# Routing rows to their experts inside the SoLU tiles instead of in a stage of its own

## The chip, the cores and the metric

One core of a Trainium2 chip runs the whole program. The time is device microseconds of one execution, median of three runs. Engines: PE (TensorE; PEld is its weight loading), ACT (ScalarE), DVE (VectorE), POOL (GpSimd), SP (SyncE, which here only issues DMAs). Each engine runs its own instructions in order; they meet at semaphores. A DMA that SP or POOL issues is carried by the core's 16 DMA engines.

## The reference, cut to what matters

```python
attn = masked_attention(q, k, v, centroids)       # 16 heads, 768 rows, head size 64
x = attn as (1536, 512)
h = x @ w_in                                      # (1536, 1024)
solu = h * softmax(h); ln = layer_norm(solu) * g_ln
x = ln @ w_out                                    # (1536, 512): the rows that are routed
logits = x @ w_gate                               # 8 experts
expert = argmax(logits); gate_w = softmax(logits)[expert]
for i in range(1536):                             # in order of the rows
    if counts[expert[i]] < 384: pos[i] = counts[expert[i]]; counts[expert[i]] += 1
out[i] = gate_w[i] * (relu(x[i] @ w1[e]) @ w2[e]) # e = expert[i]; 0 where a row found no place
```

The place of a row is its rank among the rows of the same expert, so it depends on all rows before it.

## The kernel before, in words

Four blocks follow one another, each closed by a barrier of all engines.

**Attention** (`attention`, to about 322 us): 16 heads of 6 query tiles. SP moves the next heads' operands (`load_qk`, `move_hi` with the wait of L279, `move_lo`, `move_mask`, `load_v`), one head after the other, waiting for the engines between them.

**SoLU** (`solu_block`, to about 466 us): 12 tiles of 128 rows, in software-pipelined slots (`tiles_of`). In slot i PE turns ln(i) (`turn_ln`, L129), multiplies tile i+2 into h (`up`, L121), turns x2(i-1) (L950), multiplies tile i down (`down`, L941, 24 matmuls) and multiplies x2(i-1) with the gate (`gate`, L958). ACT copies the high part of the turned ln (L885), cuts x, takes the square root for tile i+1 (L75), copies turned x2 (L878), takes the exponentials of tile i+2 (L70, with its accumulator read) and copies x2(i) out of PSUM (L900). DVE makes the low part (L917), copies the logits (L912), normalises tile i+1 (L92 to L109) and takes the maximum of tile i+2 (L79). SP stores each x2 tile to DRAM (L840). POOL cuts x and, in the first slots, expert 0's weights (L866, L868). The two x2 tiles and one PSUM bank for x2 are used in turn.

**Route** (`route`, 466 to 480 us): on all 1536 rows at once DVE makes one-hot rows, running sums over tiles, softmax weights and places; PE adds up the ranks (L1065 to L1068) and, with 12 matmuls (L1071), turns (place -> row) into `info`, for each of 24 expert tiles the row numbers and weights. DVE packs into `mask` which tiles hold rows.

**Experts** (`experts`): 8 experts with 3 token tiles each. SP loads weight pieces of 512 KB into a ring of 7. POOL gathers a tile's rows by `info` (`gather`, L1246, an indirect DMA) into one of 4 buffers and scatters results into `out` (L1260). In POOL's order gather(g+4) stands ahead of the wait for result g. PE turns the rows (L1403), multiplies up a pair of tiles (L1413), the third tile if `mask` says that it holds rows, and down (L1449).

## Time and profile before

| | us |
|---|---|
| median of 3 runs | 717.92 (714.87 to 720.31) |
| the profiled execution | 717.02 |
| its span | 715.2 |
| PE busy / DVE / ACT / POOL | 636.6 / 432.9 / 397.0 / 294.8 |
| mean granted clock of TensorE | 0.965 of full |

Starts in the timeline count from the start of the span; the execution's own time is 1.8 us above the span. Matmul ends are modelled, so starts are the safer numbers.

### The profile page before, as it was taken

How to read it: one execution, taken by the hardware profiler on the slowest of the kernel's cores; microseconds unless marked ns; L12 is line 12 of the kernel's file. 1: busy time of each engine (PE TensorE's matmuls, PEld its weight loads, DVE VectorE, ACT ScalarE, POOL GpSimd, SP SyncE). 2: the span in 40 equal slices, each digit the busy share in tenths (PEclk: the TensorE clock that was granted, in tenths of full speed). 3: DMA queues.
4: the chain of work that ended last, by engine and by line, in shares of the span. 5: the costliest groups of instructions: out<-in, count | busy, mean ns of one | idle time of the engine just before them, and what ended most of it. 6: DMA issues, size and time to landing. Idle time of an engine off the chain costs nothing. (4 is left out here: it accounts for less than half of the span.)

```text
span 715.2 us, 12775 instructions
## 1 busy us (share of the span) xinstructions
PE 636.6 (89%) x4596; PEld 570.7 (80%) x4596; DVE 432.9 (61%) x788; ACT 397.0 (56%) x671; POOL 294.8 (41%) x277
## 2 busy tenths in 40 slices
PE   2799999999999999789999998726998999999993
PEld 1799989898989899578888887615897988888982
DVE  6588888888888887356646546162563326545620
ACT  3488888887878788345454454202454335444520
POOL 3447676767876857357321000012123030341221
PEclk9999999999999999989999999956999999999997
DMA  5746565545464430073110000008666255666310
GB/s 124 214 113 155 129 159 127 141 113 150 123 163 120 111 90 2 0 245 139 45 47 26 15 30 16 29 20 292 208 210 197 83 182 192 233 206 209 110 35 12
DMA packets 37379, 86.10 MB, mean 120 GB/s; under 512 B 6719, under 2 KB 8895, under 8 KB 37314
## 3 DMA queue, kind: packets, MB, share of 16 engines
q1 hardware_dynamic: 33474, 75.78, 36.0%
q0 software_dynamic: 3840, 9.45, 3.9%
q8 instruction: 42, 0.69, 0.4%
q14 instruction: 23, 0.19, 0.1%
HBM read 53.74 MB, written 12.58 MB: 93 GB/s over the span
## 5 line engine op out<-in xcount | busy, mean ns | idle before, releaser
L557 DVE TENSOR_TENSOR p_lo<-lnt_ps,p_hi 128x384 f16<-128x384 f32 x192 | 104.6, 547 | 29.4 <-ACT p_hi L433 29.3
L433 ACT ACTIVATE p_hi<-lnt_ps 128x384 f16<-128x384 f32 x192 | 91.6, 489 | 50.7 <-PE lnt_ps L675 48.0
L552 DVE TENSOR_REDUCE neg_max<-h_ps 128x1 f32<-128x768 f32 x96 | 91.4, 952 | 20.7 <-PE h_ps L664 20.5
L675 PE MATMUL lnt_ps<-consts,p_exp 128*128 128x128 f32 x576 | 93.1, 277 | 7.6 <-DVE p_lo L557 5.7
L687 PE MATMUL one_ps<-v_cut,p_hi 128*128 128x193 bf16 x576 | 92.0, 248 | 0.7 <-ACT pv_sb L433 0.7
L664 PE MATMUL h_ps<-KK,QQ 128*128 128x384 f32 x384 | 91.9, 362 | 0.0
L1260 POOL DMA_INDIRECT out<-x_t,info x24 | 24.3, 1013 | 160.5 <-ACT x_t L1269 124.8
L688 PE MATMUL one_ps<-v_cut,p_lo 128*128 128x129 bf16 x576 | 89.5, 219 | 0.0
L455 ACT ACTIVATE p_exp<-h_ps,neg_max 128x768 f32<-128x768 f32 x96 | 86.4, 900 | 1.7 <-DVE neg_max L552 1.7
L675 PEld LDWEIGHTS lnt_ps<-consts,p_exp 128*128 128x128 f32 x576 | 69.7, 144 | 19.0 <-issue 12.7
L664 PEld LDWEIGHTS h_ps<-KK,QQ 128*128 128x128 f32 x384 | 63.4, 192 | 0.2 <-issue 0.2
L688 PEld LDWEIGHTS one_ps<-v_cut,p_lo 128*128 128x128 f16 x576 | 56.6, 98 | 1.1
L687 PEld LDWEIGHTS one_ps<-v_cut,p_hi 128*128 128x128 f16 x576 | 55.6, 96 | 1.1 <-DVE p_lo L557 1.1
L917 DVE TENSOR_TENSOR lnt_lo<-lnt_ps,lnt_hi 128x1024 fp32r<-128x1024 f32 x12 | 14.7, 1225 | 58.9 <-ACT lnt_hi L885 58.9
L352 POOL TENSOR_TENSOR qk_lo<-qk,qk_hi 128x768 fp32r<-128x768 f32 x16 | 29.3, 1830 | 49.8 <-ACT qk_hi L433 46.6
L1269 ACT ACTIVATE eht_hi<-eh_ps 128x512 fp32r<-128x512 f32 x32 | 19.2, 599 | 52.2 <-PE eh_ps L1413 48.9
L1359 DVE SCALAR_TENSOR_TENSOR eht_lo<-eh_ps,eht_hi 128x512 fp32r<-128x512 f32 x32 | 22.2, 692 | 37.1 <-ACT eht_hi L1269 34.2
L63 POOL TENSOR_TENSOR xs_lo<-x_t,xs_hi 128x512 fp32r<-128x512 f32 x12 | 15.5, 1292 | 67.0 <-ACT xs_hi L58 67.0
L1246 POOL DMA_INDIRECT x_t<-x_rows,info x24 | 33.0, 1376 | 23.6 <-issue 20.5
L1413 PE MATMUL eh_ps<-xs_hi,w_hi 128*128 128x256 f32 x128 | 37.6, 294 | 3.1 <-issue 1.7
L1269 ACT ACTIVATE x_t<-ey_ps,info 128x512 f32<-128x512 f32 x16 | 11.0, 688 | 52.8 <-PE ey_ps L1449 29.6
L941 PE MATMUL one_ps<-w_out_hi,lnt_hi 128*128 128x512 f32 x96 | 39.5, 411 | 0.0
(225 smaller groups left out, 1676.7 us busy)
## 6 DMA issues: line engine op xcount, KB each, us to landing
w_raw<-in_w SPq DMA_DIRECT2D x40, 512.0 KB, 5.1
x_t<-in_w SPq DMA_DIRECT2D x24, 512.0 KB
QQ<-qk_hi SPq DMA_DIRECT2D x32, 192.0 KB, 3.2
KK<-qk_hi SPq DMA_DIRECT2D x32, 192.0 KB, 3.7
qk<-in_qT SPq DMA_DIRECT2D x16, 192.0 KB, 3.7
qk<-in_kT SPq DMA_DIRECT2D x16, 192.0 KB, 4.4
QQ<-qk_lo SPq DMA_DIRECT2D x16, 192.0 KB, 4.0
KK<-qk_lo SPq DMA_DIRECT2D x16, 192.0 KB, 4.1
```

Source lines behind the costliest of these rows:

```text
L433: return nc.scalar.activation(out, in_, ACT.Copy, **kw)
L455: nc.scalar.activation(as_banks(p_exp[g % PX][:, :]), both(s_ps[g % 2]), ACT.Exp, bias=neg_max[:, g % PB:g % PB + 1]).then_inc(exp_done, 1)
L552: V.tensor_reduce(neg_max[:, g % PB:g % PB + 1], both(s_ps[g % 2]), AX.XY, ALU.max, negate=True).then_inc(max_done, 1)
L557: V.tensor_tensor(p_lo[g % PB][:, TH * i:TH * (i + 1), :], t_ps[i][:, 0:HALF].rearrange("p (k q) -> p k q", q=P), p_hi[g % PB][:, TH * i:T ...
L664: ins = mm(s_ps[g % 2][:, i, 0:HALF], QQ[s][:, j, P * t:P * (t + 1)], KK[s][:, j, HALF * i:HALF * (i + 1)], start=j == 0, stop=j == 1)
L675: ins = nc.tensor.transpose(t_ps[i][:, P * k:P * (k + 1)], p_exp[g % PX][:, P * kt:P * (kt + 1)], ident)
L687: mm(pv_ps[:, 0:VW], p_hi[g % PB][:, kt, :], vc[:, kt, :], start=kt == 0, stop=False)
L688: ins = mm(pv_ps[:, D:VW], p_lo[g % PB][:, kt, :], vc[:, kt, D:VW], start=False, stop=kt == T - 1)
L941: ins = mm(x2_ps[:, :], x[:, c, :], wout[w][:, c, :], start=n == 0, stop=n == 3 * FC - 1)
L1246: nc.gpsimd.indirect_dma_start(x_in[b][:, :], None, x2_dram, bass.IndirectOffsetOnAxis(ap=info[:, g, 0:1].bitcast(U32), axis=0), bounds_ch ...
L1269: return nc.scalar.activation(out, in_, func, **kw)
L1413: ins = mm(h_ps[b][:, width * i:width * (i + 1)], w[wp][:, c, P * f:P * (f + 1)], x(xp, c), start=n == 0, stop=n == 3 * KC - 1)
```

## The change

The `route` block is gone. Its work is done tile by tile in the SoLU slots, with single-tile operands of 128x8 or 128x1: `pick_expert(i-1)` on DVE at the end of slot i, `gate_exps(i-1)` on ACT ahead of the copy of x2(i), `positions(i-2)` on PE behind `turn_ln(i)` (two small bf16 matmuls into the x2 bank, which `down(i)` may not overwrite before DVE has read them), `weight_rows(i-2)` and `place_rows(i-2)` on DVE between L917 and `normalise`. The gate's matmuls stand in the middle of `down`. An x2 tile has two more columns, row number and weight, and POOL scatters its 514-column rows into a DRAM tensor sorted by expert and place (`send`), in place of SP's store. The experts then read tiles and `info` with plain loads that SP issues: four of each ahead of the weights, the later ones between weight pieces. Since unfilled places are read too, SP fills the tensor with empty rows (24 DMAs of 128 rows, two per head) during attention. `mask` is made from the last tile's counts.

```diff
 def attention(...):
+            sp.wait_ge(empty_set, 2)
             for h in range(HEADS):
...
+                for i in range(EMPTY * h, min(EMPTY * (h + 1), SLOT_TILES)):
+                    sp.dma_start(x2_dram[P * i:P * (i + 1), :], empty_row[:, :]).then_inc(filled, 16)
+            sp.wait_ge(filled, 16 * SLOT_TILES)
...
             cut_v(0)
+            Gp.memset(empty_row[:, :], 0.0).then_inc(empty_set, 1)
+            pool.wait_ge(empty_set, 1)
+            Gp.iota(empty_row[:, DM:DM + 1].bitcast(I32), ...).then_inc(empty_set, 1)
 def solu_block(...):
@@ POOL
+            def send(i):
+                s = i % 2
+                pool.wait_ge(x2_out, i + 1)
+                pool.wait_ge(weight_step, 2 * (i + 1))
+                pool.wait_ge(place_step, PLACE * (i + 1))
+                Gp.indirect_dma_start(x2_dram, bass.IndirectOffsetOnAxis(ap=place[s]..., axis=0),
+                                      x2[s][:, :], None, ...).then_inc(stored[s], 16)
+            for i in range(NT):
                 if i >= 3:
                     start.cut_x_low(pool, i, i % 2)
+                if i >= 5:
+                    send(i - 5)
+                if i < PW:
...
+            for i in range(NT - 5, NT):
+                send(i)
+            for s in range(2):
+                pool.wait_ge(stored[s], 16 * (NT // 2))
@@ ACT
+            def gate_exps(i):
+                act.wait_ge(neg_done, i + 1)
+                if not below(i, 1):
+                    act.wait_ge(weight_step, 2 * i)
+                nc.scalar.activation(ex[:, :], lg, ACT.Exp, bias=neg_lg[:, 0:1],
+                                     accum_out=total[:, 0:1]).then_inc(ex_done, 1)
@@ ACT, slot i
                     start.exps(act, i + 2, s, e_sb[:, :, :])
+                if not below(i, 1):
+                    gate_exps(i - 1)
                 act.wait_ge(x2_full, i + 1)
                 if not below(i, 2):
                     act.wait_ge(stored[s], 16 * n)
@@ DVE, six operations: maximum, ranked, best, hot16, neg_lg, base
+            def pick_expert(i): ...
@@ DVE, three operations: row number, total + 1e-9, reciprocal
+            def weight_rows(i, s, n): ...
@@ DVE, five operations
+            def place_rows(i, s):
+                dve.wait_ge(pos_full, i + 1)
+                V.tensor_tensor(mine[:, :], pos_ps, hot16[:, :], ALU.mult).then_inc(pos_read, 1)
+                V.tensor_tensor(before16[:, :], before16[:, :], hot16[:, :], ALU.add)
...
+                V.scalar_tensor_tensor(place[s][:, :], pos[:, :], base[:, 0:1], over[:, :], ALU.add,
+                                       ALU.add).then_inc(place_step, 1)
@@ DVE, slot i
                 if not below(i, 2):
-                    logits_out(i - 2)
+                    weight_rows(i - 2, s, n - 1)
+                    place_rows(i - 2, s)
                 if exists(i + 1):
                     start.normalise(...)
                 if exists(i + 2):
                     start.top(dve, i + 2, s)
+                if not below(i, 1):
+                    pick_expert(i - 1)
@@ PE, down(i)
+                if not below(i, 2):
+                    pe.wait_ge(pos_read, i - 1)
                 for c in range(FC):
+                    if c == FC // 2 and not below(i, 1):
+                        gate(i - 1)
@@ PE, turn_x2(i)
-                    pe.wait_ge(lg_out, i)
+                    pe.wait_ge(hot_done, i)
+                    pe.wait_ge(ex_done, i)
@@ PE
+            def positions(i):
+                pe.wait_ge(hot_done, i + 1)
+                pe.wait_ge(x2_out, i + 2)
...
+                ins = mm(pos_ps, tri16[:, :], hot16[:, :], start=True, stop=False)
+                ins = mm(pos_ps, ones16[:, :], before16[:, :], start=False, stop=True)
+                ins.then_inc(pos_full, 1)
             def slot(i, s, n):
                     start.turn_ln(pe, i, ln)
+                if not below(i, 2):
+                    positions(i - 2)
                 if exists(i + 2):
                     start.up(pe, i + 2, s)
...
-                if not below(i, 1):
-                    gate(i - 1)
             turn_x2(NT - 1, (NT - 1) % 2)
+            positions(NT - 2)
             gate(NT - 1)
+            positions(NT - 1)
-def route(...): ...
 def experts(...):
@@ SP
+            for g in range(XB):
+                load_x(g)
+            for g in range(XB):
+                load_info(g)
             for e in range(1, E):
                 for j in range(PW):
                     n = piece(e, j)
                     if n >= RAW:
                         sp.wait_ge(w_lo, n - RAW + 1)
                     load_expert_piece(...).then_inc(raw_in[n % RAW], 16)
+                    g = CT * e + j - (PW - CT)
+                    if j >= PW - CT and g >= XB:
+                        load_x(g)
+                        load_info(g)
@@ POOL
-            for g in range(XB):
-                gather(g)
...
             for g in range(G):
-                if g + XB < G:
-                    gather(g + XB)
                 b = g % 2
                 pool.wait_ge(y_done, g + 1)
```

## Rows read from the trace of the kernel before

**Rows 1.** Stages: attention, one SoLU slot, the placing stage. Columns in the first row.

```profile
core 0: us, PE busy (x) PEld busy (x) DVE busy (x) ACT busy (x) POOL busy (x), PEclk, DMA share, GB/s
20.00:330.00 310.00, 292.79 (x2574) 269.82 (x2574) 241.49 (x454) 232.86 (x453) 205.90 (x179) 0.99 0.48 129
387.90:401.18 13.28, 13.28 (x71) 11.15 (x70) 7.19 (x16) 6.71 (x9) 1.30 (x1) 1.00 0.05 20
470.00:480.00 10.00, 3.10 (x15) 2.85 (x15) 7.33 (x31) 0.00 (x0) 0.00 (x0) 0.50 0.00 1
```

**Rows 2.** Timeline, one SoLU slot (i=6) and the next one's start: start us, us, what.

```profile
388.22 1.03 ACT L885 ACTIVATE lnt_hi<-lnt_ps 128x1024 fp32r<-128x1024 f32 x1 [1.12 <-PE lnt_ps L129]
...
390.42 0.16 DVE L912 COPY logits<-one_ps 128x8 f32 x1
390.49 0.14 DVE L92 TENSOR_SCALAR den<-den 128x1 f32<-128x1 f32 x1
390.67 0.16 DVE L93 RECIPROCAL den<-den 128x1 f32<-128x1 f32 x1
...
393.84 0.19 PEld L941 LDWEIGHTS one_ps<-w_out_hi,lnt_hi 128*128 128x128 f32 x1
...
394.44 0.22 DVE L104 SCALAR_TENSOR_TENSOR root<-root 128x1 f32<-128x1 f32 x1
...
399.65 0.19 ACT L70 ACTIVATION_READ_ACCUMULATOR e_sb<-h_ps,neg_top 128x1 f32 x1
399.85 0.60 ACT L900 ACTIVATE x<-one_ps 128x512 f32<-128x512 f32 x1
400.27 0.94 PEld L129 LDWEIGHTS lnt_ps<-consts,ln 128*128 128x128 f32 x8
...
401.18 1.00 PEld L121 LDWEIGHTS h_ps<-w_in_hi,xs_hi 128*128 128x128 f32 x5
...
401.49 1.03 ACT L885 ACTIVATE lnt_hi<-lnt_ps 128x1024 fp32r<-128x1024 f32 x1 [1.04 <-PE lnt_ps L129]
```

**Rows 3.** Chain that ended last, from the first gather on: start us, us, what.

```profile
482.67 6.72 DMA x_t<-x_rows,info
...
491.97 12.86 PE eh_ps L1413 x96
```

**Rows 4.** Timeline, expert 2: its third token tile.

```profile
544.96 0.66 PE L1403 MATMUL ext_ps<-consts,x_t 128*128 128x128 f32 x4 [2.60 <-DMA x_t<-x_rows,info]
```

**Rows 5.** Stretches, columns as in rows 1: expert 2's first half.

```profile
541.00:566.00 25.00, 22.40 (x177) 21.80 (x175) 10.25 (x12) 9.05 (x13) 4.52 (x4) 0.93 0.50 162
```

**Rows 6.** SP's waits in attention: us in total, times, longest.

```profile
SPq L279 <- PE h_ps L664: 49.3, 14, 3.5
```

**Rows 7.** Timeline, slot 1: the operation of L104 beside POOL's weight cuts.

```profile
327.71 0.91 DVE L104 SCALAR_TENSOR_TENSOR root<-root 128x1 f32<-128x1 f32 x1
```

**Rows 8.** Timeline, the last two SoLU tiles (10 and 11).

```profile
447.11 0.58 ACT L878 ACTIVATE x2t<-one_ps 128x512 f32<-128x512 f32 x1
...
452.13 0.95 PEld L129 LDWEIGHTS lnt_ps<-consts,ln 128*128 128x128 f32 x8
...
462.20 0.60 ACT L900 ACTIVATE x<-one_ps 128x512 f32<-128x512 f32 x1 [5.01 <-PE one_ps L941]
...
463.28 0.42 PEld L950 LDWEIGHTS one_ps<-consts,x 128*128 128x128 f32 x4 [0.41 <-ACT x L900]
...
465.72 0.17 DVE L912 COPY logits<-one_ps 128x8 f32<-128x8 f32 x1 [2.56 <-PE one_ps L958]
```

**Rows 9.** Timeline, the last scatter of the kernel.

```profile
708.70 0.99 POOL L1260 DMA_INDIRECT out<-x_t,info  x1 [0.30 <-issue]
```

**Rows 10.** DMA issues: SoLU's rows to DRAM, KB each, median us to landing.

```profile
x_rows<-x SPq DMA_DIRECT2D x12, 256.0 KB, 2.0
```

**Rows 11.** Timeline, weight load of the second transpose of expert 0.

```profile
489.44 0.71 PEld L1403 LDWEIGHTS ext_ps<-consts,x_t 128*128 128x128 f32 x4 [0.39 <-DMA x_t<-x_rows,info]
```

**Rows 12.** L1246, the gathers: duration ns min/median/max of 24.

```profile
L1246 POOL DMA_INDIRECT x_t<-x_rows,info x24: 997/1274/2089, 481.1 to 683.3; - x24
```

More of the change, by code:

```diff
@@ L800, in solu_block @@
         lnt_lo = sb("lnt_lo", [P, FC, P], F32R)
-        x2 = [sb(f"x2_{s}", [P, DM], F32) for s in range(2)]
+        x2 = [sb(f"x2_{s}", [P, DM + 2], F32) for s in range(2)]
         x2t = sb("x2t", [P, KC, P], F32)
         zeros = x2[1]
+        number = sb("number", [P, NT], I32)
+        tri16 = sb("tri16", [P, P], BF16)
+        ones16 = sb("ones16", [P, P], BF16)
+        top = sb("r_top", [P, 1], F32)
+        neg_lg = sb("r_neg", [P, 1], F32)
+        ranked = sb("r_ranked", [P, E], F32)
+        best = sb("r_best", [P, 1], F32)
+        base = sb("r_base", [P, 1], F32)
+        hot16 = sb("r_hot16", [P, E], BF16)
+        before16 = sb("r_before16", [P, E], BF16)
+        ex = sb("r_ex", [P, E], F32)
+        total = sb("r_total", [P, 1], F32)
+        mine = sb("r_mine", [P, E], F32)
+        pos = sb("r_pos", [P, 1], F32)
+        over = sb("r_over", [P, 1], F32)
+        place = [sb(f"r_place{s}", [P, 1], I32) for s in range(2)]
+        held = sb("r_held", [1, E, CT], F32)
+        held_sum = sb("r_held_sum", [1, 1], F32)
         lnt_ps = start.lnt_ps
@@ L845, in _ @@
             sp.wait_ge(zeroed, 1)
-            sp.dma_start(x2_dram[NT * P:NT * P + 1, :], zeros[0:1, :]).then_inc(zeros_stored, 16)
             for t in range(NT):
-                sp.dma_start(a["out"][t * P:(t + 1) * P, :], zeros[:, :]).then_inc(zeros_stored, 16)
-            for i in range(PW - RAW):
-                store(i, i % 2)
-                load(i + RAW)
-            with sp.Fori((PW - RAW) // 2, NT // 2) as n:
-                for s in range(2):
-                    store(2 * n + s, s)
@@ L855, in _ @@
-            for s in range(2):
-                sp.wait_ge(stored[s], 16 * (NT // 2))
-            sp.wait_ge(zeros_stored, 16 * (NT + 1))
+                sp.dma_start(a["out"][t * P:(t + 1) * P, :], zeros[:, 0:DM]).then_inc(zeros_stored, 16)
+            for j in range(RAW, PW):
+                load(j)
+            sp.wait_ge(zeros_stored, 16 * NT)
         @block.gpsimd
         def _(pool):
-            nc.gpsimd.memset(zeros[:, :], 0.0).then_inc(zeroed, 1)
-            for i in range(PW):
+            Gp = nc.gpsimd
@@ new lines, in weight_rows @@
+            def weight_rows(i, s, n):
+                if not below(i, 2):
+                    dve.wait_ge(stored[s], 16 * n)
+                if below(i, 1):
+                    dve.wait_ge(constants, 1)
+                V.tensor_copy(x2[s][:, DM:DM + 1].bitcast(I32), number[:, bass.ts(i, 1)])
+                dve.wait_ge(ex_done, i + 1)
+                V.tensor_scalar(total[:, :], total[:, :], 1e-9, None, ALU.add).then_inc(weight_step, 1)
+                dve.wait_ge(weight_step, 2 * i + 1)
+                V.reciprocal(x2[s][:, DM + 1:DM + 2], total[:, :]).then_inc(weight_step, 1)
@@ L946, in turn_x2 @@
                 pe.wait_ge(x2_out, i + 1)
-                if not (isinstance(i, int) and i == 0):
-                    pe.wait_ge(lg_out, i)
+                if not below(i, 1):
+                    pe.wait_ge(hot_done, i)
+                    pe.wait_ge(ex_done, i)
                 for c in range(KC):
@@ L1492, in build @@
         consts = sb("consts", [P, width], F32)
-        logits = sb("logits", [P, NT, E], F32)
         info = sb("info", [P, E * tiles_per_expert, 2], I32)
```

311 lines of the change are left out of this document (115 added, 196 removed).

## The prediction

> **What bounds the kernel now.** I read the stretches first [rows 1]. In attention PE is busy 292.8 of 310 us with the DMA engines at a share of 0.48. In a SoLU slot PE has no idle at all: 13.28 of 13.28 us. In the ten microseconds of placing, PE has 3.1 us of work at a clock of 0.50 of full, the lower level (1.2 GHz), POOL and ACT have none, and DVE does 31 small operations: a serial stretch in which the whole core waits.
>
> Second, the timeline of a slot [rows 2] says how close the other engines are. The slot repeats after 13.27 us (L885 at 388.22 and 401.49). ACT's and DVE's round (L885, L917, normalise, maximum, exponentials, copy of x2) reaches L900 at 399.85 and ends 0.60 later, 12.23 us after it began. Only 1.04 us of it are slack. This is the number on which the SoLU part turns.
>
> Third, the chain that ended last [rows 3] goes from the placing through a gather of 6.72 us to the first matmul of expert 0 at 491.97. The weight loads were issued ahead of that gather. From then on the chain is PE's but for one place: in expert 2 PE waits 2.60 us for the third tile's gather [rows 4], which POOL issues only after a result of the expert before, and the clock then drops, to 0.93 over 25 us [rows 5].
>
> Fourth, SP in attention waits 49.3 us for PE at L279 alone, 3.5 us in each of 14 heads [rows 6].
>
> **Part 1: empty rows in attention.** Added are 24 DMAs of 263 KB, 6.3 MB, two in each of 12 heads, with an issue of some 0.5 us each. Two cost about 1 us of SP against its 3.5 us of waiting per head [rows 6], and the DMA engines are half free [rows 1]; what they delay is loaded a head ahead of its use. At 129 GB/s for a share of 0.48, full engines would carry 269 GB/s, so a fill takes 0.98 us of them. I take +0.5 us for all. Without the cover it would be 24 x 0.98 = 23.5 us; the bounds of what I believe are 0 and 3.
>
> **Part 2: the steady slot.** DVE gets eight operations between L917 and L92 in the place of one (L912). One that depends on nothing starts 0.07 after the one before (390.42, 390.49), one that waits for the last result 0.18 (390.49, 390.67) [rows 2]. Four wait (reciprocal, sum, limit, place), at 0.2; four do not, at 0.07 to 0.1; less the one removed that is +1.0 us. ACT gets a small exponential with its accumulator read: 0.20 from read to next start (399.65, 399.85) [rows 2] and 0.15 for the rest, +0.35. `pick_expert` follows the maximum and lies beside the table load and the exponentials, free. So L900 can start 11.63 + 1.35 = 12.98 us after L885, and its copy ends at 13.58; by itself this round now takes 13.6.
>
> PE gets two matmuls with 8 columns. The trace has none of that size; between 0.07 and 0.4 I take 0.2. The gate only moves. But `positions` stands right behind `turn_ln` and waits for the copy of x2, which cannot end before 1.10 us after the start of `turn_ln` (0.44 until the last matmul is out and seen, 0.60, a signal), while `up` now starts after 0.91 (400.27, 401.18) [rows 2]. The rest of a slot is 13.27 - 0.91 = 12.36. PE's own round becomes 1.10 + 0.2 + 12.36 = 13.66. The two rounds are also joined: from `turn_ln` 1.22 to L885 (400.27, 401.49) [rows 2], 13.58 to the end of the copy, 0.06, 0.2, then 12.36 to the `turn_ln` after next: 27.42 for two slots, 13.71 each. That is +0.44 in each of the eight slots 2 to 9, 3.5 us. Extra DVE time d counts half up to 0.2 and whole beyond. In slots 2 to 4 POOL cuts weights beside it, and there the operation of L104 took 0.91 for 0.22 [rows 2, 7]; half of that 0.69 in three slots is 1.0. Part 2: **+4.5 us**, from 1.6 (matmuls only, 0.2 a slot) to 8 (all eight operations at 0.18 or more).
>
> What is queued behind the new waits: behind PE's in `positions` all of `up`; behind `pos_read` in `down` nothing new, as DVE reads the ranks some 2 us ahead of `down` (393.84) [rows 2]. ACT's wait for the scatter of tile i-2: its place is known some 3.4 us after L885, POOL starts at most 0.9 later and needs 1.0 to 2.1, landing 2.0, so 8.4 at worst, 4.5 us before L900 asks.
>
> **Part 3: the last tiles, the routing's rest, the first rows.** In slot 10 turned x2 is copied at 447.11 [rows 8], behind the square root; DVE's 1.0 shifts that to 448.1, and the gate, now in the middle of `down`, waits for it. Gate 1.0 and twelve matmuls at 0.233 after 448.7 give `turn_ln(11)` at 452.6 for 452.13: +0.5. In slot 11 the gate inside `down` puts 1.0 ahead of the last copy: 463.7 for 462.20. The last transpose no longer waits for the logits' copy (463.28, where the x2 copy had ended at 462.80), so it starts at 464.4, and 2.44 later (463.28 to 465.72) [rows 8] the logits are there: 466.85. Then in series: four operations of DVE 0.8, the negative 0.1, ACT's exponential with signals 0.4, and total, reciprocal, product, sum, limit, place 1.15: 469.3. POOL starts 0.5 later and takes 0.99 [rows 9]: 470.8. The scatter's landing has no row. Plain stores land 2.0 after issue [rows 10]; behind the kernel's last scatter all that follows, landing and closing, takes 715.2 - 709.69 = 5.5. I take 2.0, between 1.0 and 5.5: 472.8. Barrier and first issue 0.5. The first rows' loads now stand ahead of the weights; two of 256 KB, 2.5 and 0.4 (between the 2.0 of [rows 10] and the 6.72 of [rows 3]): 476.2. From the second transpose to the first matmul 2.53 (489.44, 491.97) [rows 3, 11]: 478.75. The mask is made beside the scatter. So expert 0 starts 491.97 - 478.75 = **13.2 us** earlier, before part 2 is added; 5.5 with both DMAs at their upper ends, 15 with both at the lower. PE is cold in both kernels when it begins expert 0, so its 12.86 us stay.
>
> The Trainium skill, "DMA: Bandwidth & Descriptors", section "Anatomy of one DMA — SWDGE (gpsimd) path", gives 2.0 us and bytes over 436 GB/s for a DMA: an estimate of 2.6 us for the scatter and as much for a load. By that expert 0 would start 0.7 us later.
>
> **Part 4: the experts.** 24 gathers leave POOL. SP issues the rows of tile 3e+2 behind the last weight piece of expert e, which needs only that the first piece of e has been cut, early in expert e-1: a lead of most of an expert. So the wait of 2.60 [rows 4] goes, and with it the drop of the clock, 0.07 x 25 = 1.75 [rows 5], of which I take 1.4: **-4.0 us**, between 0 and -4.35. The 24 small DMAs more (8 bytes a row) run where the queue is not the limit.
>
> **Sum** on the profiled execution of 717.0: +0.5 + 4.5 - 13.2 - 4.0 = -12.2, **704.8 us**. The median shown is 0.9 higher, inside the spread of its three runs (714.9 to 720.3); I keep 705.
>
> **The rivals.**
> *The slot pays more.* If the small operations with their waits cost 0.3 each rather than 0.07 to 0.2, DVE's round grows by 2.3 and a slot takes 14.6: 8 x 1.33 = 10.6 for 4.5, 711. For it: 1.04 us of slack is all there is. Against it: the spacing in [rows 2] already has such waits. Chance 0.13.
>
> *POOL and DVE hinder one another.* Each slot now has a scatter at POOL while DVE normalises. In this trace the same instruction form took from 997 to 2089 ns beside DVE [rows 12], and L104 0.69 more beside POOL [rows 7]. If each send holds DVE as L104 was held, a slot takes 13.60 + 0.69 = 14.29 for 13.71: 0.58 in slots 5 to 9 and 0.2 more in slots 2 to 4, which already pay for L104, some 3.5 us, 708.5. Against it: L104 was held beside copies and subtractions of 128x1024 tiles (L866, L868), not beside an indirect DMA. Chance 0.12. The Trainium skill, "SBUF — State Buffer", section "SBUF: two separate sides", says that the port pair shared by DVE and GpSimd is locked for a whole instruction and that DVE can keep GpSimd from writing descriptors; by that the delay falls on the sends, where the 4.5 us of part 2 hide it. The trace agrees with a lock in one direction at least: 2089 against 997.
>
> *The first rows stay late.* Scatter 5.5 and load 6.72 in place of 2.0 and 2.5: 7.7 us less, 712.5. For it: a load of rows took that long in [rows 3]. Against it: the weights stood ahead there. Chance 0.10.
>
> *Slower: the fills are not hidden.* Attention is the longest stage and PE fills 94% of it. If the 6.3 MB stand in the queue ahead of operands that the next head waits for, each costs up to 0.98: 24 x 0.98 = 23.5 for 0.5, 728. It decides from 0.5 us per fill. Against it: the half-free engines and SP's 3.5 us. Chance 0.05.
>
> **How the numbers follow.** The forecast has 0.60, the rivals 0.13, 0.12, 0.10 and 0.05. A measurement of this kernel tells about 1% from no change; faster by over 1% is below 710.7. The forecast's own range is 700 to 709, the low end where the DMAs land at once and the slots pay 0.2 each; taking in the three middle rivals gives 699.5 to 712. Faster: nearly all of the forecast, most of the second rival and half of the first, 0.77. Slower 0.05, the rest 0.18.
>
> **What would show it.** Right: a slot period near 13.7 with PE waiting a few tenths ahead of the small matmuls; some 9.6 us from the last copy of x2 to the first DMA of the experts (463.7 to 473.3 above), 2 of them the scatter's landing; the first matmul of expert 0 some 8 us earlier than 491.97 (13.2 less 4.5 and 0.5); no wait of PE for rows in expert 2 and a clock of 1.00 there; attention of the same length to within 1 us. Wrong: slots of 14.3 or more, a first row load over 5 us, new PE waits for weights in experts 0 and 1, or an attention longer by more than 3 us.

## The result and the profile after

| | before | after | ratio |
|---|---|---|---|
| median of nine runs, us | 718.95 (714.87 to 720.31) | 712.85 (711.22 to 716.09) | 0.992 [0.990, 0.994] |
| the same kernel again, beside eleven runs of before, us | 718.49 | 711.68 | 0.990 [0.987, 0.993] |
| span of the profiled execution, us | 715.2 | 714.3; again 710.0 | |

The change makes the kernel 6 to 7 us faster; the forecast was 12 to 13. The execution profiled first was the slowest of its nine, so I use the second profile of the same kernel ("again") beside it. In both, the time splits at three places that every profile shows: the first `turn_ln` (L129), the `turn_ln` of the last tile, and expert 0's first matmul.

| stretch, us | before | after | after again | change, again | forecast |
|---|---|---|---|---|---|
| start to first `turn_ln` | 305.63 | 307.35 | 307.29 | +1.7 | +0.5 |
| eleven slot periods | 146.64 | 157.58 | 154.86 | +8.2 | +5.0 |
| last `turn_ln` to expert 0's first matmul | 39.71 | 30.78 | 29.22 | -10.5 | -13.7 |
| from there to the end | 223.2 | 218.6 | 218.6 | -4.6 | -4.0 |
| sum | 715.2 | 714.3 | 710.0 | -5.2 | -12.2 |

Attention took 1.2 us more than forecast (experiment 5), the experts 0.6 less; 3.2 us are missing in the slots and 3.2 behind them. A slot's period, from its `turn_ln` to the next, says where:

| period from `turn_ln` of tile | 0 | 1 | 2 | 3 | 4 | 5 | 6 | 7 | 8 | 9 | 10 |
|---|---|---|---|---|---|---|---|---|---|---|---|
| before | 14.86 | 13.55 | 13.27 | 13.27 | 13.27 | 13.27 | 13.27 | 13.27 | 13.27 | 13.27 | 12.07 |
| after again | 14.51 | 13.49 | 13.75 | **17.28** | 13.83 | **15.04** | 13.73 | 13.83 | 13.48 | 13.49 | 12.43 |

The plain slots stand near the forecast 13.71. Two are 3.5 and 1.2 us longer than their neighbours, and they are so in both profiles (17.27 and 15.10 in the first). Of the forecast's signs of being right, one fails at once: expert 0's first matmul was to come some 8 us before 491.97, and it comes at 491.37, in the first profile at 495.71. Of its signs of being wrong, slots of 14.3 us or more are there, but two of them only.

The stretches of the first profile of after, with the columns of [rows 1]: attention, one plain slot, expert 2's first half.

```profile
core 0: us, PE busy (x) PEld busy (x) DVE busy (x) ACT busy (x) POOL busy (x), PEclk, DMA share, GB/s
20.00:330.00 310.00, 292.87 (x2567) 270.38 (x2567) 241.37 (x449) 230.33 (x450) 205.03 (x180) 0.99 0.56 152
386.00:399.50 13.50, 13.50 (x71) 11.07 (x70) 8.52 (x26) 6.85 (x11) 2.29 (x2) 1.00 0.05 19
541.00:566.00 25.00, 24.51 (x188) 23.02 (x186) 11.92 (x13) 11.53 (x16) 3.98 (x3) 1.00 0.60 198
```

Against [rows 1] the DMA share of attention rises from 0.48 to 0.56 and PE's busy time does not move (292.79, 292.87). In expert 2 [rows 5] the clock is back at 1.00 and PE is busy 24.5 us instead of 22.4.

The timeline around the long period of tile 3, which begins at 349.30. POOL splits the weights for expert 0 into a high part (CAST) and a low part (the subtraction of L917); these are its cuts (first profile of after: start us, us, engine, line, operation; in brackets the idle time before it and what ended it):

```profile
342.25 1.05 POOL L915 CAST w_hi<-w_raw 128x1024 fp32r<-128x1024 f32 x1
...
343.39 2.39 POOL L917 TENSOR_TENSOR w_lo<-w_raw,w_hi 128x1024 fp32r<-128x1024 f32 x1
...
343.91 1.89 DVE L104 SCALAR_TENSOR_TENSOR root<-root 128x1 f32<-128x1 f32 x1
...
347.41 1.23 DVE L79 TENSOR_REDUCE neg_top<-h_ps 128x1 f32<-128x1024 f32 x1
...
348.73 1.28 ACT L70 ACT_TABLE_LOAD   x1 [4.63 <-DVE neg_top L79]
...
350.02 1.11 ACT L70 ACTIVATE e_sb<-h_ps,neg_top 128x1024 f32<-128x1024 f32 x1
...
351.13 0.26 ACT L935 ACTIVATE r_ex<-one_ps,r_neg 128x8 f32<-128x8 f32 x1
...
351.37 0.59 ACT L959 ACTIVATE x<-one_ps 128x512 f32<-128x512 f32 x1
...
352.24 0.18 PE L1085 MATMUL one_ps<-r_hot,tri 128*128 128x8 bf16 x1 [1.90 <-ACT x L959]
```

Read from the bottom. PE waits 1.90 us for ACT's copy of x2 (L959). That copy stands behind the exponentials (L70, L935), these behind a table load (ACT_TABLE_LOAD: ACT changes from the square root's table to the exponential's), and the table load starts only when DVE's maximum (L79) has ended. The maximum is late because L104, an operation on 128x1 elements that takes 0.22 us elsewhere, took 1.89. It ends at 345.80, within 0.02 us of POOL's subtraction (343.39 + 2.39 = 345.78). In the kernel before, the same pair stands in another place and I had seen only half of it [rows 7]:

```profile
326.22 2.39 POOL L868 TENSOR_TENSOR w_lo<-w_raw,w_hi 128x1024 fp32r<-128x1024 f32 x1
```

It ends at 328.61, L104 at 327.71 + 0.91 = 328.62. So L104 is not slowed by some share; it waits for the rest of POOL's instruction. I call the time above its usual 0.22 the hold. The change put the scatter (1.0 to 1.2 us) ahead of the weight cuts on POOL, and with that more of the subtraction over L104: in slots 2, 3 and 4 it is held 1.67, 1.34 and 1.33 us, where the kernel before had 0.46, 0.50 and 0.52 (and 0.69 in slot 1). PE asks for the copies behind them in slots 3, 4 and 5. In slot 4 PE, itself late by then, does not wait. The other DVE operations beside that subtraction (L100 and L103, one tensor each) took their usual 0.15 and 0.16.

Behind the wait in slot 3 the granted clock falls to 0.59 of full for a stretch. The first eight matmuls of `up` take 3.38 us there and 2.10 in a plain slot. The row of that stretch in the profile of after again, columns as above:

```profile
352.10:355.50 3.40, 3.39 (x11) 2.61 (x11) 2.62 (x12) 2.37 (x3) 1.28 (x1) 0.59 0.00 0
```

The last tiles and the first rows, timeline of the profile of after again:

```profile
472.82 0.60 ACT L959 ACTIVATE x<-one_ps 128x512 f32<-128x512 f32 x1 [1.57 <-PE one_ps L1056]
...
477.05 0.27 ACT L935 ACTIVATE r_ex<-one_ps,r_neg 128x8 f32<-128x8 f32 x1 [2.29 <-DVE r_neg L979]
...
478.27 0.22 DVE L1003 SCALAR_TENSOR_TENSOR r_place<-r_pos,r_base,r_over 128x1 int32<-128x1 f32 x1
...
479.36 0.98 POOL L902 DMA_INDIRECT x_sorted<-x,r_place  x1 [2.51 <-DVE r_place L1003]
484.48 2.77 SPq L1193 DMA_DIRECT2D x_t<-x_sorted  x4
484.78 0.98 POOL L1220 MEMSET x_t<- 128x512 f32 x2 [4.45 <-POOLq L803]
...
487.98 1.57 PEld L1370 LDWEIGHTS ext_ps<-consts,x_t 128*128 128x128 f32 x8 [10.79 <-DMA x_t<-x_sorted]
...
491.36 0.29 PEld L1380 LDWEIGHTS eh_ps<-xs_hi,w_hi 128*128 128x128 f32 x1 [1.81 <-DVEq L1167]
```

From the last send's end (480.34) to the first row load are 4.14 us (3.80 in the first profile), where I had put 2.5; from the load's issue to the first matmul 6.88, where I had put 5.4. From the end of the last copy of x2 (473.42) to the first row load are 11.1 us, where the forecast's sign was 9.6.

### The profile page after: what moved, and what is told of

The parts are those of the page before. It is cut to its first block and busy times, and to the rows that moved or that the text cites. A ratio compares the mean times of both kernels' runs of the same rounds, so it can differ in the third digit from the quotient of the medians.

```text
span 714.3 us, 12985 instructions
## 1 busy us (share of the span) xinstructions
PE 643.0 (90%) x4607; PEld 573.9 (80%) x4607; DVE 448.7 (63%) x902; ACT 398.5 (56%) x694; POOL 276.0 (39%) x242
## 5 line engine op out<-in xcount | busy, mean ns | idle before, releaser
L1226 POOL DMA_INDIRECT out<-x_t,info x24 | 27.3, 1136 | 193.4 <-ACT x_t L1235 142.8
L1056 PE MATMUL one_ps<-w_out_hi,lnt_hi 128*128 128x512 f32 x96 | 41.6, 433 | 4.6 <-DVE r_mine L996 4.6
L1056 PE MATMUL one_ps<-w_out_lo,lnt_hi 128*128 128x512 f32 x96 | 39.5, 411 | 0.0
L1056 PE MATMUL one_ps<-w_out_hi,lnt_lo 128*128 128x512 f32 x96 | 39.4, 410 | 0.0
```

Of the source, the lines that this page charges most:

```text
L1056: ins = mm(x2_ps[:, :], x[:, c, :], wout[w][:, c, :], start=n == 0, stop=n == 3 * FC - 1)
```

## The experiments

The edits are made in the kernel after where nothing else is said; each kernel is timed beside the kernel before on the same chip. "Wait" is idle time of PE in the profile.

**1. The kernel after, again.**

> The changed kernel once more, nothing edited. The record has it at 712.85 (0.9917 of before), while the profiled execution took 716.09, the slowest of nine. Theory A (POOL's weight cuts hold DVE's L104 for 1.9 and 1.6 us in slots 2 and 4, so PE stalls in slots 3 and 5): the two long slots come back at the same places, 1.9 and 1.3 us of PE idle, since nothing in them is left to chance. Theory B (the long slots are chance, from a clock that drops): L104 near 0.7 and at most one long slot. What is chance in either is the clock: the 1.9 us that attention lost at 28 to 33 us and the slow matmuls of slots 3 and 10 may be gone, 2 to 5 us together.

711.68 us, ratio 0.990 [0.987, 0.993]. L104's three durations recur within 0.01 us (1.90, 1.56, 1.55), and the two long periods within 0.06. The first profile's period of tile 10 (15.00) does not: it is 12.43 here. There PE waited 1.55 us for the copy of turned x2, here 0.37, and the clock granted over the period was 0.80 of full there and 0.86 here; the matmuls behind the wait took 0.63 instead of 0.40 us.

**2. The weights cut ahead of the send.**

```
 for i in range(NT):
-    if i >= 5:
-        send(i - 5)
     if i < PW:
         ... the two cuts of piece i ...
+    if i >= 5:
+        send(i - 5)
```

> POOL cuts weight pieces 5, 6 and 7 ahead of the scatter of their slot and not behind it. Theory A: the long subtraction then ends before L104 is due, L104 is back at 0.22, the PE stalls of slots 3 and 5 go (3.2 us, and up to 1.9 more where the clock would have dropped): 3 to 5 us less than the unedited kernel of the same call. Theory B: no more than 1 us of difference. Rival C (the scatters themselves hold DVE): L104 stays above 0.5 in slots 6 to 10 too.

708.60 us, ratio 0.985 [0.979, 0.990]. The timeline of POOL in this kernel, same stretch:

```profile
342.48 2.39 POOL L915 TENSOR_TENSOR w_lo<-w_raw,w_hi 128x1024 fp32r<-128x1024 f32 x1
345.04 1.20 POOL L902 DMA_INDIRECT x_sorted<-x,r_place  x1 [0.17 <-issue]
```

The subtraction now ends before L104 starts, and from slot 2 on L104 takes 0.22. The periods of tiles 3 and 5 fall from 17.28 and 15.04 to 14.46 and 14.13, together 3.7 us, while the total falls by 3.1 (medians). Not all is gone: PE's waits of 0.69 and 0.38 stay in those two periods. The edit did not only take a hold away, it made another. POOL's first cut now lies over DVE's last operation of `place_rows`, which also reads two tensors:

```profile
341.36 1.04 POOL L913 CAST w_hi<-w_raw 128x1024 fp32r<-128x1024 f32 x1
...
341.73 0.68 DVE L1003 SCALAR_TENSOR_TENSOR r_place<-r_pos,r_base,r_over 128x1 int32<-128x1 f32 x1
```

It ends at 342.41, the cut at 342.40, and in the slots without cuts it takes 0.22: slots 2, 3 and 4 are held 0.46 us each on the same round.

**3. Turned x2 copied ahead of the square root in slot 10.**

```
 early = i == NT - 2
+if early: x2t_out_of(i - 1)
 if exists(i + 1): start.square_root(act, i + 1)
-if not below(i, 1): x2t_out_of(i - 1)
+if not below(i, 1) and not early: x2t_out_of(i - 1)
```

> In slot 10 ACT copies turned x2(9) ahead of the square root of tile 11, so that the gate in the middle of the multiplication down need not wait for DVE's normalisation. Theory: slot 10 took 15.0 us for 12.07 before because PE waits 1.55 us for that copy in the middle and 2.2 us for DVE ahead of it, and runs the rest at the lower clock; without the first wait 13 to 13.5, so 1.5 to 2 us less than the unedited kernel. Rival: the clock drops from the 2.2 us wait alone; then only the 1.5 us wait goes and the low stretch stays, 0.5 to 1 us less in all.

711.75 us, ratio 0.989 [0.984, 0.994]. The period of tile 10 falls from 12.43 to 10.46 in the profile, and the four profiles with this edit (experiments 3, 4, 11 and 12) have 10.14 to 10.46 where the other kernels with the change have 12.28 to 15.00. Most of that goes with the clock: the wait for the copy was 0.37 us in the profile of after again, and the granted clock over the period is 0.86 there and 1.00 here. The median does not show the gain (711.68 and 711.75), as the spread of eight runs is 5 us. ACT's queue in that slot, of this kernel:

```profile
450.32 0.59 ACT L928 ACTIVATE x2t<-one_ps 128x512 f32<-128x512 f32 x1
...
450.93 1.28 ACT L75 ACT_TABLE_LOAD   x1
...
456.07 0.20 ACT L75 ACTIVATE root<-root 128x1 f32<-128x1 f32 x1 [3.86 <-DVE root L100]
```

The copy had stood behind a square root that waits 3.9 us for DVE, and the gate inside `down` behind the copy. In the long periods nothing changed (17.31 and 15.16): the two effects are separate.

**4. Three edits: experiments 2 and 3, and the ranks read ahead of number and weight.**

```
 def weight_rows(i, s, n):
+    dve.wait_ge(pos_full, i + 1)
+    V.tensor_tensor(mine, pos_ps, hot16, ALU.mult).then_inc(pos_read, 1)
+    V.tensor_tensor(before16, before16, hot16, ALU.add)
     V.tensor_copy(x2[s] number column, number of tile i)
 ...
 def place_rows(i, s):
-    dve.wait_ge(pos_full, i + 1)
-    ... the same two operations ...
```

> Both edits of the runs beside it, and DVE reads the ranks (mine, before16) ahead of the row number and the weight, so that the multiplication down of slots 10 and 11 can start 0.3 us earlier. If the three prices add up: 3 to 5, 1.5 to 2 and 0.6, so 5 to 7 us less than the unedited kernel, about 706. If the clock only moves its low stretch to another gap: 3 to 4 us less.

703.77 us, ratio 0.979 [0.974, 0.984]. Ahead of `down` in slots 10 and 11 PE waits 1.92 and 1.54 us, where it waited 2.23 twice; the period of tile 10 is 10.15.

**5. The fills alone, on the kernel before.**

```
+for i in range(EMPTY * h, min(EMPTY * (h + 1), SLOT_TILES)):
+    sp.dma_start(spare[P * i:P * (i + 1), :], empty_row[:, :]).then_inc(filled, 16)
```

> The kernel before plus only the 24 stores of an empty row per tile that the change puts on SP's queue during attention (here into a spare tensor that nothing reads; memset without the iota, and one word narrower in nothing). Theory: they lie beside attention's compute and cost nothing, ratio to before 0.998 to 1.002 (my forecast's part 1 said +0.5 us). Rival (fills not hidden): each loads SP's queue and the DMA engines ahead of a q, k or v piece, and attention ends 10 us or more later: 728 us or more. The 1.7 us by which the changed kernel's profiled attention was longer arose within 28 to 33 us, where the transposes ran at 0.90 instead of 0.55 us; if the fills cause it, it is here too: +1.7 us, ratio 1.0024.

719.24 us against 719.18, ratio 1.001 [0.998, 1.003]. The first `turn_ln` is at 305.51, before without fills at 305.63. In its row for attention only the last two columns, DMA share and GB/s, differ from [rows 1] by more than 1%:

```profile
20.00:330.00 310.00, 292.54 (x2576) 270.12 (x2577) 242.12 (x454) 232.31 (x453) 207.28 (x180) 0.99 0.56 150
```

The fills cost nothing that the runs can resolve. Where the +1.7 us of attention in two profiles of after come from stays open. In the ten profiles of kernels with the whole change attention ends at 305.4 to 305.6 five times and at 307.0 to 309.4 five times; in the late ones PE gets through 21 to 29 matmuls from 28 to 33 us, in the others 42 to 47. The four profiles of kernels without the new routing, this one among them, are not late (304.8 to 305.6); that is too few to call it chance or effect.

**6. The gathers issued two tiles earlier, on the kernel before.**

```
+gather(XB); gather(XB + 1)
 for g in range(G):
-    if g + XB < G: gather(g + XB)
+    if g + XB + 2 < G: gather(g + XB + 2)
```

> The kernel before with one edit in the experts: each gather of rows is issued two tiles earlier on POOL's queue (two more ahead of the loop, then gather g+XB+2 at tile g instead of g+XB), so that it no longer queues behind a scatter that waits for a late tile. Theory (part 4 of my forecast: the wait of 2.60 us of expert 2's first rows and the cold clock behind it are what the experts gain): -2.6 to -4.6 us against before, ratio 0.9936 to 0.9964, and the wait of 2.60 at 544.96 is gone. Rival (the experts' gain of the changed kernel comes from the plain loads themselves, or from chance in the clock): no gain, ratio 0.999 to 1.001. A second rival: the buffer that the gather fills is only free later, so the earlier issue waits at the head of POOL's queue and the scatters behind it are late: slower by 1 us or more.

717.08 us, ratio 0.997 [0.994, 0.999]: -2.1 us by the medians and -3.3 by the spans of the profiles (711.6 for the 714.9 of experiment 5). In the place of [rows 4] stands this row of the timeline, and the row of the stretch of [rows 5] is as in the kernel after:

```profile
542.52 0.63 PE L1405 MATMUL ext_ps<-consts,x_t 128*128 128x128 f32 x4 [0.49 <-issue]
```

```profile
541.00:566.00 25.00, 24.51 (x210) 23.90 (x209) 10.25 (x12) 9.06 (x13) 5.34 (x4) 1.00 0.48 162
```

So the wait of 2.60 and the clock behind it were the gather's place in POOL's queue, and a small edit of the kernel before takes them away without the new routing. It accounts for 3.3 of the 4.6 us that the experts gained in the profiles of after; the other 1.3 are not isolated.

**7. The first rows loaded behind six weight pieces.**

```
-for g in range(XB): load_x(g)
-for g in range(XB): load_info(g)
 for e in range(1, E):
     for j in range(PW):
         n = piece(e, j)
+        if n == RAW - 1:
+            ... the same eight loads ...
```

> The changed kernel with one edit: SP issues the experts' first four row loads (and number and weight) behind the first six of expert 1's weight pieces (0.5 MB each) instead of ahead of them. In the kernel before, POOL's gathers of the first rows ran beside those pieces and took 6.72 us. Theory: what the changed kernel gains at the first rows (3.53 us of load instead of 6.72) is in good part the order: six pieces of 0.5 MB at the rate that the queue shows take 6 to 8 us, and the first matmul of expert 0 comes 6 to 9 us later than unedited (slot 11 to it: 35 to 39 us instead of 29.2), the ratio to before 0.998 to 1.004. Rival (the load's time is its own latency, the DMA engines serve queues side by side): +2 us or less, all of it SP's issue time, ratio 0.990 to 0.993.

722.47 us, ratio 1.006 [1.004, 1.008]; from the last `turn_ln` to the first matmul 37.18 us for 29.22. SP's queue in this kernel, and PE's wait:

```profile
486.29 2.34 SPq L777 DMA_DIRECT2D w_raw<-in_w  x4
488.67 2.05 SPq L779 DMA_DIRECT2D x_t<-in_w  x2
490.77 2.32 SPq L1193 DMA_DIRECT2D x_t<-x_sorted  x4
...
498.36 0.90 PE L1371 MATMUL ext_ps<-consts,x_t 128*128 128x128 f32 x3 [18.80 <-DMA x_t<-x_sorted]
```

SP's issues of the six pieces delay the loads by 4.5 us, and the loads then take 7.6 instead of 3.5. Together these make 8.0 us more from the last `turn_ln` to the first matmul (37.18 for 29.22), most of what the kernel loses against the unedited one (10.8; attention was 2.1 longer in this profile). So with the rows behind the weights the changed kernel is 3.3 us slower than before: its gain hangs on the order in SP's queue. This profile shows one thing more. L104 took 1.89, 1.57 and 1.55 us as before, but the granted clock stayed at 1.00, and the periods of tiles 3, 4 and 5 are 15.65, 14.67 and 14.74, with waits of PE of 1.90, 0.93 and 0.98. So of the 3.5 us of slot 3 some 1.6 belong to the clock, and the second hold, which reached no wait of PE in slot 4 there, costs 0.93 here. The three periods together are 45.1 us for 46.2.

**8. The SoLU slots written out.**

```
 def tiles_of(eng, n_tiles, slot):
-    for s in range(2): slot(s, s, 0)
-    with eng.Fori(1, n_tiles // 2 - 2) as n:
-        for s in range(2): slot(2 * n + s, s, n)
-    for i in range(n_tiles - 4, n_tiles): slot(i, i % 2, i // 2)
+    for i in range(n_tiles): slot(i, i % 2, i // 2)
```

> The changed kernel with one edit: the SoLU block's twelve slots written out for every engine instead of two, a hardware loop of three rounds over two, and four. Theory: in the loop a slot takes 13.73 to 13.83 us and outside, where nothing else waits, 13.48; that 0.25 to 0.3 us is waiting on register values by the engines that form the slot's chain, so written out slots 2 to 7 lose 0.25 each, -1.5 us in all, ratio to before about 0.988. Slots 3 and 5 stay long (about 17.2 and 15.0), since POOL's piece beside VectorE's small operation is unchanged. Rival: the 0.25 us belongs to the weight pieces that POOL cuts in these slots, and stays: ratio 0.990; or the longer code is fetched late and makes slots longer than 13.8.

706.53 us, ratio 0.984 [0.980, 0.988], where the unedited kernel has 0.990 [0.987, 0.993]: 5.2 us by the medians, known only to within some 4 us, and 6.0 in the slots of the profiles, from an edit for which I had expected 1.5. The plain slots fall to 13.5, as expected. What I had not expected is that the long ones go too, to 13.93 and 13.67, although L104 takes as long as before (1.89, 1.57, 1.56). The timeline of this kernel, the counterpart of the one above:

```profile
342.94 0.58 ACT L923 ACTIVATE x2t<-one_ps 128x512 f32<-128x512 f32 x1
343.54 1.28 ACT L70 ACT_TABLE_LOAD   x1
347.75 1.12 ACT L70 ACTIVATE e_sb<-h_ps,neg_top 128x1024 f32<-128x1024 f32 x1 [2.93 <-DVE neg_top L79]
```

```profile
343.33 1.89 DVE L104 SCALAR_TENSOR_TENSOR root<-root 128x1 f32<-128x1 f32 x1
...
346.50 1.22 DVE L79 TENSOR_REDUCE neg_top<-h_ps 128x1 f32<-128x1024 f32 x1
```

The table load now stands right behind ACT's last copy, four microseconds before the maximum is there. In the loop it came behind the maximum. The trace of before shows the same two orders, inside the loop and outside it:

```profile
397.34 1.28 ACT L70 ACT_TABLE_LOAD   x1 [2.59 <-DVE neg_top L79]
...
421.30 1.28 ACT L70 ACT_TABLE_LOAD   x1
423.73 1.12 ACT L70 ACTIVATE e_sb<-h_ps,neg_top 128x1024 f32<-128x1024 f32 x1 [1.14 <-DVE neg_top L79]
```

So a slot in the loop has 1.28 us less of slack on the round of ACT and DVE. That order is shown. That it is what shortens the long slots is argued: it would leave 0.6 of the 1.92 us of waiting in slot 3, and 0.27 are there, but writing out also takes the loop's register instructions away, and no run separates the two. Why the loop has the other order (in the loop the wait is against a register's value, outside against a constant) is my reading of the code.

**9. The kernel before, written out.**

> The kernel before with its twelve SoLU slots written out. In its trace the exponentials' table load of 1.28 us follows the maximum in the loop (397.34, after neg_top at 396.02 + 1.23) and comes ahead of it outside (421.30, where neg_top starts at 422.47), yet slots take 13.27 either way, since PE bounds them. Theory: no change, ratio 0.998 to 1.002: the table load's place costs only where the round of ACT and VectorE is the longer one, as in the changed kernel, where writing the slots out gave 5.2 us. Rival: written-out code is faster by itself (no register waits): 6 slots x 0.25 = 1.5 us or more, ratio 0.998 or less.

720.32 us, ratio 1.001 [0.997, 1.005]; its slots stay at 13.26 and 13.27, although L104 took up to 1.48 and the table load now stands ahead of the wait. Where PE alone bounds the slot, neither the table load's place nor the hold costs anything. This is the control for experiment 8. (In this profile the way from the last `turn_ln` to expert 0 is 3.1 us longer than before; the medians, 720.32 beside 719.31, do not resolve it.)

**10. L104 with one tensor.**

```
-V.scalar_tensor_tensor(root[:, 3:4], root[:, 0:1], root[:, 2:3], root[:, 1:2], ALU.mult, ALU.add)
+V.tensor_scalar(root[:, 3:4], root[:, 0:1], root[:, 2:3], root[:, 1:2], ALU.mult, ALU.add)
```

> The changed kernel with one edit: L104 (a 128x1 operation of VectorE that reads two tensors and one scalar per partition from SBUF, 0.22 us) becomes a tensor_scalar that reads one tensor and two scalars per partition, same values. In every slot in which L104 started beside POOL's subtraction of 2.39 us it ended within 0.02 us of that subtraction's end (before: 340.66+... 342.04 and 342.06, 355.35 and 355.36; changed: 345.57 and 345.59), while VectorE's operations with one tensor ran on beside it in their usual time. Theory: VectorE's operations with two tensors from SBUF wait for POOL's instruction to end, those with one do not; so the new operation takes 0.15 to 0.2 in all slots, slots 3 and 5 fall from 17.3 and 15.0 to 13.8, and the time is 711.7 - 3.5 - 1.2 = 707, ratio to before 0.984. Rival: whatever stands in that place beside POOL's subtraction is held, and the time stays at 711.7, ratio 0.990.

709.17 us, ratio 0.984 [0.979, 0.990]. All twelve instances take 0.27 or 0.28, also beside POOL's subtraction. The timeline of this kernel, DVE and then POOL:

```profile
342.31 0.27 DVE L104 TENSOR_SCALAR root<-root 128x1 f32<-128x1 f32 x1
342.62 0.15 DVE L105 TENSOR_SCALAR root<-root 128x1 f32<-128x1 f32 x1
...
343.25 1.50 DVE L109 TENSOR_SCALAR ln<-z,mv,root 128x1024 f32<-128x1024 f32 x1 [0.28 <-DVE root L106]
```

```profile
341.80 2.40 POOL L917 TENSOR_TENSOR w_lo<-w_raw,w_hi 128x1024 fp32r<-128x1024 f32 x1
```

The small operations from L104 to L106 run beside POOL's instruction, held by nothing. The next one, L109, has 128x1024 elements and takes 1.50 instead of 0.81: it starts inside the subtraction, which ends at 344.20, and 0.69 of the 1.67 us moved there. It ends 0.55 us after the subtraction. That is no coincidence: in the thirty instances of L109 over all profiles that took over 0.9 us, it ends 0.54 to 0.56 us after the end of a POOL instruction, however long it took (up to 2.60). The long periods are 14.75 and 14.12, with waits of 0.99 and 0.38.

The size does not settle it. In slot 1 of this kernel an operation on 128x8 elements, with one tensor and one scalar of each partition and a bf16 result, waits as long as any; it takes 0.23 elsewhere, and it ends at 333.61, the subtraction at 333.57:

```profile
331.18 2.39 POOL L917 TENSOR_TENSOR w_lo<-w_raw,w_hi 128x1024 fp32r<-128x1024 f32 x1
...
331.87 1.74 DVE L978 TENSOR_SCALAR r_hot<-r_ranked,r_best 128x8 bf16<-128x8 f32 x1
```

So "any operation in that place is held" has fallen, and "only those with two tensors" as well. Held are operations with two tensors from SBUF, whatever their size, and some with one; the one-tensor operations on 128x1 elements were not.

**11. The first rows' loads issued inside the SoLU block**, on the kernel of experiment 4.

```
     sp.wait_ge(zeros_stored, 16 * NT)
+    for s in range(2): sp.wait_ge(stored[s], 16 * (NT // 2))
+    for g in range(len(x_in)):
+        sp.dma_start(x_in[g], x2_dram rows of tile g).then_inc(x_here[g], 16)
```

> The kernel of the three edits (weights cut ahead of the send, turned x2 copied ahead of the square root in slot 10, ranks read ahead of number and weight) plus one: the experts' first four row loads are issued by SP at the end of the SoLU block, as soon as the scatters have landed, so that the barrier between the blocks lies beside them. Between the end of POOL's last send and SP's first row load lie 3.8 to 4.1 us in the changed kernel, where I forecast 2.5. Theory: about 2 us are the scatter's landing and about 2 the barrier and the blocks' entries, so the first row load is issued 1.5 to 2.2 us earlier after POOL's end, and the time is 702 us, 1.5 to 2.2 below the three edits' 703.8; ratio to before 0.976. Rival: the landing takes 3.5 us of the 3.8 and the barrier hardly anything: no gain, 703.8, ratio 0.979, and the row load still starts 3.5 us or more after POOL's end.

703.87 us, ratio 0.977 [0.972, 0.981]. POOL's queue and SP's, of this kernel:

```profile
472.25 0.97 POOL L907 DMA_INDIRECT x_sorted<-x,r_place  x1 [2.36 <-DVE r_place L1011]
```

```profile
475.55 1.76 SPq L896 DMA_DIRECT2D x_t<-x_sorted  x4
```

From the send's end to the load 2.33 us instead of 3.80 in experiment 4's profile: so 2.3 are the scatter's landing and its signal up to SP's issue, 1.5 the barrier and the blocks' entries. Over the seven profiles with the loads first behind the barrier the way is 3.60 to 4.14, so the barrier's part is 1.3 to 1.8. Expert 0 starts 1.1 us earlier after the last `turn_ln` (27.16 for 28.24). By the medians (703.87 and 703.77) the gain is not resolved.

**12. All edits together** (4, 8, 10 and 11).

> All edits together: the three, the row loads at the end of the SoLU block, the twelve slots written out, and L104 made an operation that reads one tensor (the other two as scalars of each partition). Theory: the gains add where they touch different waits. Written out, slots 2 to 7 take 13.5 instead of 13.75 to 14.5: the three edits' kernel has 84.6 us in slots 2 to 7, 81 would be 3.6 less; with the loads' 1.5 to 2.2 that gives 698 to 699, ratio to before 0.970 to 0.973. Rival: the slots' gains overlap with those of the edits already in it, or the longer code costs what it gives: 702 or more.

700.06 us (698.51 to 701.75), ratio 0.971 [0.967, 0.975]: 19 us below before, more than twice what the change itself brings. Slots 2 to 9 take 13.49 to 13.53, and PE's waits in them are gone. The periods of tiles 2 to 7 are together 3.1 us shorter than in experiment 4, which is most of the 3.7 us between the medians.

## Why the prediction was wrong

**Part 1, the fills: right.** +0.5 forecast, +0.1 measured, between -1.1 and +2.3 (experiment 5); the rival that they are not hidden, 23 us, fell with it.

**Part 2, the plain slot: right for the loop.** DVE's eight operations cost 1.1 us (forecast 1.0), ACT's exponential 0.25 (0.35), the two matmuls together 0.21 (0.2). The period is 13.73 to 13.83 in the loop against 13.71; outside it 13.48, which is PE's own round (13.27 + 0.21). I had read ACT's round from [rows 2], where the table load stands between maximum and exponentials, and took that for a property of the slot. It is one of the loop.

**Part 2, L104 beside POOL: the step that failed first.** The prediction priced it as "half of that 0.69 in three slots is 1.0". Two slots came out 3.5 and 1.2 us long, and taking the hold of L104 away gives 2.8 and 0.9 of that back (experiment 2): 3.7 us for the 1.0. Three things were wrong in it. The 0.69, which is slot 1's (slots 2 to 4 of before had 0.46 to 0.52), was what happened to be left of POOL's instruction when L104 started, not a price: two rows of before, laid side by side, end within 0.01 us of each other and say so. The edit moved POOL's cuts by a send, so what was left grew to 1.67. And the half that I took for hidden was not there: the slack of [rows 2], 1.04 us, had already been spent by part 2 itself, so nearly all of it reached PE (a wait of 1.90). Behind that wait came a stretch of low clock, for which the prediction had no term in the slots; it is some 1.6 us of the 3.5 (experiment 7).

The rival "POOL and DVE hinder one another" named the place, but priced a send holding DVE, and no DVE operation was held beside a send; L104's four holds in the trace before are all beside subtractions (L868), none beside a copy, where the prediction named both. The Trainium skill, "SBUF — State Buffer", section "SBUF: two separate sides", states the condition that I had not applied: a DVE instruction in a 2-port mode, or one with two SBUF inputs beside a GpSimd instruction that reads SBUF, contends for a port pair shared by the two engines, and the one that starts second waits until the other has ended. The rows here agree: L104 with two inputs was held by a subtraction that reads SBUF (1.67 us), with one input it was not (experiment 10). L109 (0.69) and L978 (1.51), with one input, were held too; whether they ran in a 2-port mode no row here shows.

**Part 3, the last tiles: right in sum.** The last send was to start 17.2 us after the last `turn_ln`; it started at 479.36 - 462.15 = 17.2. The wait of 2.23 us ahead of `down` in the last two slots, which it left unsaid, did not disturb the sum, as the kernel before had waits of 2.54 and 2.61 in the same two slots for the logits' copy. That the copy behind the square root costs 2 us there, which one edit gives back (experiment 3), it did not see.

**Part 3, send to first matmul: the step that failed second.** The prediction's 2.0 for the scatter's landing and 0.5 for barrier and first issue measured 4.14: the landing 2.3 and the barrier 1.3 to 1.8 (experiment 11). Its 2.5 and 0.4 for the loads, then 2.53 to the first matmul, measured 6.88: the load took 3.50 until the first transpose, and the transposes and cuts 3.38. The sum is 11.0 for 7.9. I had taken the landing from a plain store, and the barrier from nothing: no row stands behind the 0.5. The rival "the first rows stay late" came nearer by its time (712.5) than by its mechanism, since neither DMA took the 5.5 and 6.72 that it gave them. What the prediction held against it, that the weights had stood ahead in [rows 3], experiment 7 bears out: behind them the load takes 7.6.

**Part 4, the experts: right.** -4.0 forecast, -4.6 measured in both profiles; experiment 6 isolates the wait and the clock behind it, with -2.1 in the medians and -3.3 in the spans.

So of the 7 us between forecast and result, 3.2 are in the slots (the two long ones 3.7 above what was put for the hold, the two plain ones outside the loop 0.5 below), 3.1 in the stretch from send to first matmul, 1.2 are in attention, whose cause is open, and the experts gave 0.6 back.

What stays open: experiment 2 keeps waits of 0.69 and 0.38 us in periods 3 and 5 with L104 free, experiment 4 of 0.72 and 0.43. DVE's last operation of `place_rows` is held in the slots ahead of them, 0.46 us each in experiment 2 and 0.16 in experiment 4 (where the addition of L997, moved forward, is held 0.5 us), and written out the waits are gone, so they lie on the same round of ACT and DVE. Why slots 3 and 5 show them and slot 4 does not was not isolated.

## What to carry to other kernels

Before work is put ahead of something on one engine's queue, look at what its instructions overlap on the other engines: where a small operation is far above its usual time, compare its end with the ends of its neighbours, and if they coincide, price the rest of the neighbour, from where the small operation will start. When an edit moves the neighbour away, look at what it lies over now. The slack of a round is spent once; every further delay then counts in full, and a cost that was free in the kernel before (a hold, a table load behind a wait) is on the path in the kernel after. And read a slot inside the hardware loop and one outside it: where their order differs, writing the loop out may be worth as much as the change.

## What the runs showed of the hardware

- A DVE operation of 128x1 elements with two tensors from SBUF waited up to 1.67 us for the end of POOL's subtraction and ended 0.01 or 0.02 us after it; the same values from one tensor and two scalars took 0.27 or 0.28 always. The addition of L997, two tensors of 128x8, took 0.34 in the middle of its twelve instances and 0.15 at least: beside POOL's cut of x in the profile of after again (353.26 and 1.28 long) it ended 0.02 us after it.
- A one-tensor operation can be held as well: L109, 128x1024 from SBUF to SBUF, took up to 2.60 us for 0.81 and ended 0.54 to 0.56 after POOL's instruction in thirty instances; L978, 128x8 to bf16, took up to 1.74 for 0.23. L94, of the same size as L109 but with one of its two tensors in PSUM, took its 1.28 beside the same subtraction (experiment 2, 342.71).
- In the hardware loop the exponentials' table load (1.28 us) comes behind the wait for their operand, in written-out code ahead of it. Writing out was worth 5.2 us by the medians in the kernel after, and nothing in the kernel before (1.001 [0.997, 1.005]).
- After an indirect scatter of 128 rows of 2 KB, SP's next load was issued 2.3 us after POOL's instruction ended where it waited for the scatter alone; the barrier between two blocks with the entry into the next took another 1.3 to 1.8 us.
- The first of four 256 KB row loads let PE start 3.0 to 3.6 us after its issue with nothing ahead of it, and 7.6 us behind six weight pieces of 0.5 MB.
